# Spreading the first loads over two DMA queues, freeing the last chunk's output place, and reordering the casts of the first layer run in an attention + two-MoE-layer kernel

## The reference

```python
# attention: batch 4, heads 8, seq 768, head_dim 64
state = gamma * state + k_t v_t^T            # per head, gamma = 1 - 2^(-5-h)
y_t   = (1/sqrt(64)) * q_t @ state
x = y as 3072 tokens x 512 features
# layer 1: w_in 512 x 2048, w_out 2048 x 512
h = relu(x @ w_in);  x = (h*h) @ w_out
# layer 2: w_gate, w_val 512 x 1536, w_out 1536 x 512
xn = x / sqrt(mean(x*x) + 1e-6) * rms_g
out = (silu(xn @ w_gate) * (xn @ w_val)) @ w_out
```

## Time and profile before

| | us |
|---|---|
| median of 3 runs | 1072.89 |
| lowest, highest | 1072.64, 1073.95 |
| the profiled execution | 1074.1 |
| its span (first to last instruction) | 1072.3 |
| PE busy in the span | 1063.3 (99%) |
| ACT busy, DVE busy, POOL busy | 622.0, 874.9, 332.4 |
| DMA moved | 195.85 MB, 183 GB/s on average |

### The profile page before, as it was taken

The page is one execution under the profiler, slowest core; times in us unless marked ns, Lnnn a source line. Parts: engine busy times, 40 slices in busy tenths (PEclk is TensorE's granted clock), DMA queues, the critical chain, the costliest instruction groups (busy, mean ns, idle before and its releaser), DMA issues.

```text
span 1072.3 us, 15713 instructions
## 1 busy us (share of the span) xinstructions
PE 1063.3 (99%) x5971; PEld 893.6 (83%) x5971; DVE 874.9 (82%) x939; ACT 622.0 (58%) x911; POOL 332.4 (31%) x242
## 2 busy tenths in 40 slices
PE   8999999999999999999999999999999999999998
PEld 7887788888888888888888888888888888888898
DVE  5695999878879878889889998987886986978684
ACT  3886776467665567664674555646455555444353
POOL 1763542003550005530025554005544102544000
PEclk9999999999999999999999999999999999999999
DMA  9999458763446654455653235632225751130455
GB/s 351 372 405 408 185 214 291 238 218 119 156 177 226 206 178 154 161 223 193 213 171 106 96 141 201 213 136 71 68 62 143 270 194 59 47 111 20 141 187 184
DMA packets 80586, 195.85 MB, mean 183 GB/s; under 512 B 24160, under 2 KB 34528, under 8 KB 75648
## 3 DMA queue, kind: packets, MB, share of 16 engines
q1 hardware_dynamic: 78160, 190.55, 51.6%
q10 hardware_dynamic: 2352, 4.31, 1.1%
HBM read 152.26 MB, written 42.48 MB: 182 GB/s over the span
## 4 chain that ended last, share of the span: by engine, by line
PE 95%; DMA 2%; DVE 1%; ACT 1%; issue 1%; SPq 0%; ACTq 0%; DVEq 0%
PE Y L841 13%; PE Y L843 13%; PE Y L842 13%; PE Z L841 8%; PE X L841 8%; PE Z L843 8%; PE X L843 8%; PE X L842 8%; PE Z L842 8%; DMA item_scratch<-ops 2%; PE Z L787 1%; PE Z L777 1%; PE Y L762 1%; PE X L762 1%; PE R L807 1%
## 5 line engine op out<-in xcount | busy, mean ns | idle before, releaser
L686 POOL TENSOR_TENSOR w_ops<-raw_w,w_ops 128x512 fp32r<-128x512 f32 x90 | 128.0, 1422 | 489.8 <-ACT w_ops L968 489.6
L1028 ACT CAST ops<-hid 128x1024 fp32r<-128x1024 f32 x147 | 154.7, 1053 | 162.9 <-PE Z L843 55.1
L1407 DVE TENSOR_TENSOR ops<-hid,ops 128x1024 fp32r<-128x1024 f32 x147 | 179.9, 1225 | 45.5 <-ACT ops L1028 45.1
L686 POOL TENSOR_TENSOR w_ops<-sums_w,w_ops 128x512 fp32r<-128x512 f32 x120 | 167.2, 1396 | 128.0 <-ACT w_ops L968 127.6
L841 PE MATMUL Y<-ops,w_ops 128*128 128x512 f32 x360 | 140.4, 390 | 2.5 <-ACT u L1058 1.7
L843 PE MATMUL Y<-ops,w_ops 128*128 128x512 f32 x360 | 140.1, 389 | 0.0
L842 PE MATMUL Y<-ops,w_ops 128*128 128x512 f32 x360 | 140.1, 389 | 0.0
L1067 ACT ACTIVATE gt<-gt 128x512 f32<-128x512 f32 x72 | 45.1, 632 | 111.5 <-DVE gt L1624 38.9
L843 PE MATMUL Y<-ops 128*128 128x512 f32 (+1 forms) x288 | 104.4, 363 | 0.0
L841 PE MATMUL Y<-ops 128*128 128x512 f32 (+1 forms) x288 | 104.4, 363 | 0.0
L842 PE MATMUL Y<-ops 128*128 128x512 f32 (+1 forms) x288 | 104.4, 363 | 0.0
(11 more groups left out here) (175 smaller groups left out, 2347.8 us busy)
## 6 DMA issues: line engine op xcount, KB each, us to landing
ops<-item_scratch SPq DMA_DIRECT2D x147, 512.0 KB, 3.8
raw_w<-w_f SPq DMA_DIRECT2D x30, 1024.0 KB, 5.1
item_scratch<-hid SPq DMA_DIRECT2D x30, 512.0 KB, 3.1
qk_sb<-qkv SPq DMA_DIRECT2D x24, 512.0 KB, 8.9
kv_sb<-qkv SPq DMA_DIRECT2D x20, 512.0 KB, 9.5
y_scratch<-hid SPq DMA_DIRECT2D x12, 512.0 KB, 5.9
raw<-y_scratch SPq DMA_DIRECT2D x3, 2048.0 KB, 10.2
raw<-w_b SPq DMA_DIRECT2D x5, 1024.0 KB, 5.0
```

The lines of the kernel that those rows point to most:

```text
L686: nc.gpsimd.tensor_tensor(w_ops[:, k, 1], front_w_source(m, k), f32(w_ops[:, k, 0]), ALU.subtract).then_inc(w_lo, 1)
L1028: nc.scalar.copy(hop_at(n)[:, 0], hid[:, 2 * g:2 * g + 2, OPERAND[k], :]).then_inc(hop_hi, 1)
L1407: nc.vector.tensor_tensor(hop[:, 1], hid[:, 2 * g:2 * g + 2, OPERAND[k], :], f32(hop[:, 0]), ALU.subtract).then_inc(hop_lo, 1)
```

## The change

Three edits, all in the first 110 us or so. (1) SP issues qk0 ahead of the tables, and kv0 and kv1 go out on ACT's queue, behind the decay rows; SP's order is then qk0, tables, qk1, qk2, kv2, qk3, kv3, kv4. (2) Chunk 23's output is copied to place 0 of `qk_sb`, free by then, and no longer waits for a store of `y_sb`; the wait for all `x_stored` moves from `save_u2` of run 0 to the start of run m = 1. (3) In run 0 alone, `prep` casts the activation operand ahead of the next run's weight block.

```diff
+            load_qk(0)
             sp.dma_start(tables_sb[:], tables).then_inc(tables_loaded, 16)
-            load_qk(0)
             load_qk(1)
-            load_kv(0)
-            for n in range(2, QKR):
+            load_qk(2)
+            for n in range(3, QKR):
+                load_kv(n - 1)
                 load_qk(n)
-                load_kv(n - 1)
             load_kv(QKR - 1)
             load_kv(QKR)
@@ copy_out
-                if i >= 3:
+                place = qk_sb[:, 0, QT, :] if n == NCH - 1 else y_sb[:, i % 3, :]
+                if 3 <= i and n < NCH - 1:
                     act.wait_ge(x_stored[i % 3], 16 * (i // 3))
-                nc.scalar.copy(y_sb[:, i % 3, :], Z[:, n % 2, :]).then_inc(y_copied, 1)
+                nc.scalar.copy(place, Z[:, n % 2, :]).then_inc(y_copied, 1)
@@ save_u2
-                if run == 0:
-                    for i in range(3):
-                        act.wait_ge(x_stored[i], 16 * len(stored_chunks()[i::3]))
@@ front_run of ACT
                 def prep(slot):
-                    if more and slot:
+                    if more and slot and m:
                         high_w(m + 1, slot - 1)
                     if fresh and slot < 4:
                         high_front(front, 3 + slot)
+                    if m == 0 and slot:
+                        high_w(1, slot - 1)
...
+                if m == 1:
+                    for i in range(3):
+                        act.wait_ge(x_stored[i], 16 * len(stored_chunks()[i::3]))
@@ start of ACT's program
             act.dma_start(staged_rows[0:4 * H], decay_rows).then_inc(rows_loaded, 16)
+            for n in range(2):
+                act.dma_start(kv_sb[:, n], qkv[0, n, :, 2:, :]).then_inc(kv_loaded[n], 16)
```

More of the change, by code:

```diff
@@ L937, in copy_out @@
                 i = stored_chunks().index((b, c))
-                if i >= 3:
+                place = qk_sb[:, 0, QT, :] if n == NCH - 1 else y_sb[:, i % 3, :]
+                if 3 <= i and n < NCH - 1:
                     act.wait_ge(x_stored[i % 3], 16 * (i // 3))
-                nc.scalar.copy(y_sb[:, i % 3, :], Z[:, n % 2, :]).then_inc(y_copied, 1)
+                nc.scalar.copy(place, Z[:, n % 2, :]).then_inc(y_copied, 1)
                 act.wait_ge(y_copied, n + 1)
-                act.dma_start(x_dram[i].rearrange("p h k t -> p (h k t)"), y_sb[:, i % 3, :])\
+                act.dma_start(x_dram[i].rearrange("p h k t -> p (h k t)"), place)\
                     .then_inc(x_stored[i % 3], 16)
```

## The result

The changed kernel takes 1071.41 us (median of 19 runs, 1070.81 to 1073.21), the kernel before, in the 19 runs that stand for it now, 1073.43 (1072.5 to 1074.53). The ratio is 0.9983, with a 95% interval of 0.9976 to 0.9990: lower by 2.0 us. The interval leaves out 1, so a gain is shown, though it is smaller than the 0.2% (2.15 us) within which the prediction called two times the same. The profiled execution took 1070.97, its span is 1069.2; before, 1074.1 and 1072.3.

What follows compares the result with a forecast made beforehand. PE was taken as the bound, busy without a break after 111 us, so only its earlier stops counted: 0.95 + 1.01 + 0 - 0.55 = 1.4 us, from 1072.89 to 1071.5; own range 1070.9 to 1072.2, 8 in 10 1070.0 to 1073.3.

Steps and rivals of the forecast that it cites:

- part 1: First loads: qk1 delayed to 11.4 by shared DMA engines, attend(0) at 12.6, 0.75 later; net loss 0.55 us.
- Part 3, first stop: Run 0, PE's wait before product 4: `save_u2` comes 0.95 us earlier, so the stop shrinks from 1.85 to 0.90.
- The hold between DVE and POOL: Run 0: DVE and POOL operations hold each other; with POOL's block later, the first sum moves 0.1 to 0.2 at most.
- E: Rival: item stores land later, operand k = 5 waits past 100.5, copy not earlier; about 1073 us, chance 0.07.
- Part 3, second stop: Run 0, PE's wait before product 6: goes entirely, 1.01 us, with nothing in hand; bounds 0.2 and 1.01.
- Rival C: The stop before product 6 stays at 0.8 us because POOL holds DVE again; 1072.3 us, chance 0.13.
- Part 2: Last chunk's copy released about 0.9 us sooner, but ACT reaches the same later waits: 0 us, at most 0.9.
- rival B: At the start, queues take turns by whole transfers, so qk1 comes at 10.1, attend(0) 0.4 earlier; 1070.5 us, chance 0.27.
- D: Rival, slower: tables come too late behind qk0, attend(0) at 14.4, 2.55 later; 1074.3 us, chance 0.08.

Runs made afterwards that it cites:

- run 0: Not a follow-up run: the kernel's front run 0, whose first product (L915) starts at 90.69 us before and 89.62 us in the changed kernel.
- casts: The kernel before with only the casts' order in run 0 changed (operand cast ahead of the weight cast): 1071.9 us, ratio 0.9986.
- noloads: The changed kernel with the old order of the loads: 1071.74 us, ratio 0.9981.
- again: The changed kernel once more, with no edit: 1071.82 us, ratio 0.9982.
- noplace: The changed kernel with the last chunk's output back in `y_sb` and the waits for the stores back in `save_u2`: 1071.33 us, ratio 0.9977.
- u2first: The changed kernel with `save_u2` right behind operand k = 5 and the relu of X ahead of the third weight cast: 1070.94 us, ratio 0.9976.
- kvact: The kernel before with kv0 and kv1 on ACT's queue, the tables still first: 1072.61 us, ratio 0.9994.
- warm: The kernel before with seven products on zeros in PE's wait for qk0: 1073.3 us, ratio 0.9999.
- u2old: u2first with the old order of the loads, on SP's queue alone: 1070.83 us (five runs), ratio 0.9968.
- loads: The kernel before with only the loads' order changed (qk0 first, kv0 and kv1 on ACT's queue): 1073.48 us, ratio 1.0001.

## Why the prediction was right where it was, and wrong where it was not

- **Forecast and time.** The forecast was 1071.5, the measured time is 1071.41. From its own base each is a gain: 1.4 forecast, 2.0 measured. The 0.6 between them is the loss that I had put on part 1. That the two times agree to 0.1 is luck: the kernel before measured 1073.43 in these runs and not 1072.89, and this 0.5 hides the loss that did not come.
- **Part 3, first stop: right.** From the cast of k = 3 to `save_u2` it was 7.85, forecast 6.9; measured 6.91 (94.03 to 100.94). The stop is 0.75 shown, as forecast. The hold between DVE and POOL moved, as the argument said, and did not delay the first sum. The hold fell on the low part instead of the combine, with the same end. Two of the signs that I had named failed: ACT's idle ahead of the cast from `sums_w` is 2.00 and not below 1, and there is none ahead of operand k = 5. Both come from item 9 (see E below), and neither moves the copy, which the sum decides.
- **Part 3, second stop: right.** It is gone, in every trace with the new order (casts, noloads, again, noplace, changed). I had called this the softest term: L1610, the old L1605, ends at 107.17, 0.44 before product 6 starts at 107.61, so there was some slack where my count had none. Rival C is out.
- **Part 2: right.** The copy starts 0.88 sooner against L915 and ACT waits 1.21 for product 0. noplace is level.
- **Part 1: wrong, in sign.** I had written that I am wrong if attend(0) starts before 11.85, and it starts at 10.81. The step that failed is "by the time qk0, tables and qk1 (1124 KB) are through, the decay rows, kv0 and kv1 (1136 KB) are too: 2260 KB", put at 11.4, hence attend(0) at 12.6. Its first half, even turns, holds. The DMA view of the changed kernel from 7 to 8 us has both queues at work alike (q1 is SP's, q10 ACT's: packets, MB, share of 16 engines):

```profile
q1 hardware_dynamic: 52, 0.21, 51.7%
q10 hardware_dynamic: 51, 0.21, 50.7%
```

And qk1 and kv1 land within 0.2 to 0.3 of each other (9.72 and 10.03 here; u2first 9.45 and 9.75; noplace 9.62 and 9.82), where rival B wanted kv1 a transfer behind qk1: 512 KB at 420 GB/s are 1.2 us. kvact has them 0.75 apart (8.82 and 9.57).

What failed is the time of the 2260 KB. I took it from the old landings, as if 1748 KB had been all that was out when kv0 landed at 10.6. The DMA view of the kernel before up to 10.6 us, and below it that of the changed kernel up to 9.72, show more, and the same in both:
```profile
DMA packets 873, 2.72 MB, mean 257 GB/s; under 512 B 101, under 2 KB 229, under 8 KB 873
...
DMA packets 868, 2.72 MB, mean 280 GB/s; under 512 B 96, under 2 KB 224, under 8 KB 868
```

At kv0's landing 0.9 MB of the loads behind it had moved already, so the 2.5 us per MB that I worked out from landings was no price of the bytes ahead. It was also one execution's: with the same loads in the same order POOL got kv0 at 10.61, 10.43, 10.07, 9.66 and 9.38 (before, warm, noloads, u2old, casts). Last, I read a busy share of 0.89 as engines with nothing to spare. From 8 to 10 us they moved 279 and 332 GB/s before, and 418 and 418 now, at shares of 1.03 and 1.02; casts moved 295 at a share of 1.07. attend(0) comes earlier than in the trace of before, not later, in all five traces of kernels with the changed loads (10.81, 11.27, 11.34, 10.72, 10.54).
- **And it does not show in the time.** By the profiles the loads give 0.5 to 1.1; loads measured 1.0001, and noloads and again lie 0.1 apart. The scatter of the start explains a part: attend(0) in the traces with the old loads is 11.07 to 11.85 but for one at 9.57, so the trace of before was a late one. The late stop of 0.2 to 0.5 between 833 and 837 us takes a part in some executions (again has it, the first profile of the same kernel not). I had named any stop after 111 us as a sign that I am wrong. The profile of the changed kernel has none, 7 of the 12 others have this one. Whether an earlier PE makes it more likely is only an argument: kvact, with the earliest run 0, has none, and no run tests it.
- **Rivals.** B's time of 1070.5 was reached by neither median of this kernel (1071.41, 1071.82), though its early attend(0) came true, by another mechanism. The Trainium skill's rule on which it leaned ("DMA: Bandwidth & Descriptors", section "Queues, rings and completion order": a whole packet is drained before the engine goes to the next queue) may hold for packets smaller than these transfers; no run here shows such a case. For turns by whole transfers the landings of qk1 and kv1 speak against it. D is out: the tables are there at 6.61 for the mask. E is out: operand k = 5 was cast at 97.36. Item 9's store, issued at 78.7, took 18.3 us and landed at 97.0, 7.4 after L915, where I had counted 8.8 (99.5 less 90.69). It was 0.3 us ahead of the cast.

That last point is a second slip, without a price here: I carried the items' landings over as if they kept their distances to run 0. In the chain of waits of the changed kernel item 7's store, which the earlier trace rows have at 17.39, took 16.09, and operands k = 4 and 5 were cast without a wait:
```profile
77.44 16.09 DMA item_scratch<-ops
```
In u2first operand k = 5 did wait for its item, till 98.17. That is 8.81 after L915, the distance that I had forecast, so the store can bound a further step in that direction.

What stays open: why the engines move 360 to 434 GB/s in each microsecond from 8 to 10 in all five traces in which qk0 goes first and kv0 and kv1 go on the second queue, while in the others, with one of the two edits or none, one microsecond at least stands at 332 or less; and what decides between 1.16 and 2.08 for scores(0).

## What to carry to other kernels

Where PE is busy without a break behind a certain point, count only the stops ahead of that point. An operation that has its input can be moved into another engine's idle wait, ahead of the copy that PE stands for; that takes about its length off the stop (0.95 forecast, 0.94 measured here), as long as what ends the wait keeps its time. Ask for every microsecond won at the start which later load or store it runs into, and do not price a start from one profiled execution: here it varied by 1 us and more, as much as the edit could give. The next step in run 0, in u2first, was to make the copy before the cast that waits, and not only to fill the wait. Don't read the price of a byte off the time at which a load landed: later loads may have been moving beside it.

## What the hardware showed that I had not expected

- The share of busy time of the DMA engines is no measure of free capacity: 0.89 went with 279 and 332 GB/s, 1.02 and 1.03 with 418, and 1.07 with 295 (casts, 8 to 9 us).
- A load's landing is no count of the bytes moved: when kv0 landed at 10.6, 1748 KB (1.79 MB) had been issued up to and with it, and 2.72 MB had moved.
- Sixteen equal matmuls of scores(0) took 1.16, 1.24, 1.54 or 2.08 us at the same place, in two executions of one program too (1.16 and 2.08). Only the 1.54 went with a granted clock below 1.00 in the rows (0.83, then 0.50). In both kernels that kept PE busy with zeros past qk0's landing it was 1.16, but it was that in some kernels without them too, so no run shows that the zeros did it.
- Two queues with large transfers shared the engines evenly: 52 and 51 packets, 0.21 and 0.21 MB, from 7 to 8 us, and two 512 KB loads that began near each other landed 0.2 to 0.3 us apart in three traces, 0.75 in a fourth. With small packets of the tables on one of them the count was near even and the bytes were not: 78 and 88 packets, 0.07 and 0.36 MB, from 5 to 6 us.
